# A fused mixing layer with two MLPs, its main loop unrolled: softmax weights in two buffers and a phase earlier, and the leaky layer as a parametric ReLU in place in PSUM

## The reference

```python
w = softmax(weight_gen, axis=-1)             # (2, 4096, 8 heads, 7 taps)
x_pad = concatenate([zeros(6 rows), x])      # causal, per batch
out[s, h] = sum_k w[s, h, k] * x_pad[s + k, h]     # 24 features a head
h = out @ w_in;  g = maximum(0.01 * h, h)    # leaky layer, 192 -> 2048
x2 = g @ w_out                               # 2048 -> 192
h = x2 @ w_in2;  g = where(h > 0, h, exp(minimum(h, 0)) - 1)   # ELU layer
return g @ w_out2
```

## Time and profile before

| | |
|---|---|
| median of the runs | 1238.52 us |
| the profiled execution | 1236.35 us |
| its span, first to last instruction | 1234.6 us |
| TensorE busy (9808 matmuls) | 1156.0 us, 94% |
| VectorE busy | 828.8 us, 67% |
| ScalarE busy | 740.3 us, 60% |
| GpSimd busy | 486.8 us, 39% |
| mean granted TensorE clock | 0.976 |

### The profile page before, as it was taken

The page is one execution under the profiler, slowest core; times in us unless marked ns, Lnnn a source line. Parts: engine busy times, 40 slices in busy tenths (PEclk is TensorE's granted clock), DMA queues, the critical chain, the costliest instruction groups (busy, mean ns, idle before and its releaser), DMA issues.

```text
span 1234.6 us, 24425 instructions
## 1 busy us (share of the span) xinstructions
PE 1156.0 (94%) x9808; PEld 1007.4 (82%) x9808; DVE 828.8 (67%) x817; ACT 740.3 (60%) x846; POOL 486.8 (39%) x411
## 2 busy tenths in 40 slices
PE   7698998989989899898989989899898989989998
PEld 4576887878889888787878889899787878889986
DVE  6969775756757567575765757567575766756564
ACT  3455756656665565656656565565656656565674
POOL 5919054270824609054180723609145180730000
PEclk9999999999999899899999999899899999999999
DMA  6220112010120200212011120200202001110000
GB/s 173 65 84 27 62 40 63 25 57 16 38 61 25 74 13 25 61 34 65 25 40 34 38 61 25 70 14 28 61 25 74 25 21 52 38 25 27 14 27 27
DMA packets 44651, 54.39 MB, mean 44 GB/s; under 512 B 4116, under 2 KB 32914, under 8 KB 44624
## 3 DMA queue, kind: packets, MB, share of 16 engines
q1 hardware_dynamic: 44624, 54.01, 14.5%
HBM read 36.29 MB, written 17.69 MB: 44 GB/s over the span
## 4 chain that ended last, share of the span: by engine, by line
PE 86%; issue 5%; DVE 4%; POOL 4%; ACT 1%; DMA 1%; SPq 0%; POOLq 0%
PE y_a_rows L617 27%; PE hidden L549 27%; PE y_b L610 19%; PE hidden L553 9%; PE hidden L578 4%; DVE hid_lo L1116 1%; POOL mix L323 1%; POOL prod L311 1%; PE hidden L579 1%; DVE act L1086 1%; DMA xw<-in_x_dram 1%; DVE up_b_lo L998 0%; DVE act L1089 0%; POOL prod L336 0%; DVE up_a_lo L988 0%
## 5 line engine op out<-in xcount | busy, mean ns | idle before, releaser
L617 PE MATMUL y_a_rows<-hid_hi,dn 64*128 64x512 f32 x2048 | 577.0, 394 | 0.0
L1116 DVE TENSOR_TENSOR hid_lo<-act,hid_hi 128x1024 fp32r<-128x1024 f32 x255 | 338.5, 1328 | 217.0 <-ACT hid_hi L908 217.0
L610 PE MATMUL y_b<-hid_hi,dn 64*128 64x512 f32 x1024 | 403.3, 394 | 50.4 <-issue 46.5
L610 PE MATMUL y_b<-hid_lo,dn 64*128 64x512 f32 x1024 | 400.3, 391 | 0.0
L617 PEld LDWEIGHTS y_a_rows<-hid_hi,dn 64*128 64x128 f32 x2048 | 339.8, 188 | 26.6
L617 PE MATMUL y_a_rows<-hid_lo,dn 64*128 64x512 f32 x1024 | 355.8, 392 | 0.0
L908 ACT ACTIVATE hid_hi<-act 128x1024 fp32r<-128x1024 f32 x255 | 268.3, 1052 | 1.7 <-DVE act L1089 1.5
L311 POOL TENSOR_TENSOR mix<-xw,wk 128x384 f32<-128x384 f32 x30 | 27.1, 904 | 579.9 <-DVE wk L1026 577.0
L893 ACT ACTIVATE act<-hidden 128x1024 f32<-128x1024 f32 x127 | 130.5, 1027 | 204.4 <-PE hidden L553 162.5
L610 PEld LDWEIGHTS y_b<-hid_hi,dn 64*128 64x128 f32 x1024 | 192.1, 188 | 72.5 <-issue 54.3
L311 POOL TENSOR_TENSOR prod<-xw,wk 128x384 f32<-128x384 f32 x180 | 243.3, 1358 | 9.4
(11 more groups left out here) (105 smaller groups left out, 1109.5 us busy)
## 6 DMA issues: line engine op xcount, KB each, us to landing
xw<-in_x_dram SPq DMA_DIRECT2D x14, 960.0 KB
raw_b<-squares_out SPq DMA_DIRECT2D x60, 96.0 KB, 2.2
out_dram<-staged SPq DMA_DIRECT2D x15, 384.0 KB, 2.3
squares_in<-prod SPq DMA_DIRECT2D x56, 96.0 KB, 4.5
squares_out<-ya SPq DMA_DIRECT2D x15, 256.0 KB, 2.0
raw_a<-squares_in SPq DMA_DIRECT2D x14, 256.0 KB, 2.9
raw_d<-in_moe_w_out_dram SPq DMA_DIRECT2D x8, 384.0 KB, 4.2
raw_a<-in_moe_w_in_dram SPq DMA_DIRECT2D x8, 256.0 KB, 4.1
```

The lines of the kernel that those rows point to most:

```text
L610: return nc.tensor.matmul(y_b[:, :], dn[m][rows, f, P:2 * P], v[rows, s % HB, HALF[i]], start=start, stop=stop)
L617: return nc.tensor.matmul(bank[:, :], dn[m][rows, f, first:first + P], v[rows, s % HB, HALF[i]], start=(f == 0 and n == 0), stop=(f == FT ...
L1116: nc.vector.tensor_tensor(hid_lo[:, s % HB, :], act[:, s % 2, :], hid_hi[:, s % HB, :].bitcast(f32), ALU.subtract).then_inc(s_lo, 1)
```

## The change

1. The hardware loop is gone: all 32 phases are written out for each engine.
2. The softmax weights have two buffers, and the softmax of chunk c+3 is done in the ELU phase of chunk c (`softmax_a` after step 3, `softmax_exp` after step 4, `softmax_b` after step 5), where it was that of chunk c+1 in the leaky phase of chunk c. That is one phase earlier for each chunk. `turn_mix` goes from step 1 to step 2, behind `add_y`, and the leaky input from steps 4 and 5 to 5 and 6.
3. The leaky step is one parametric ReLU on ScalarE, from `hidden` to `hidden`. Rounding reads `hidden` in the same step; VectorE's rest reads `hidden` too, and the maximum on VectorE is gone. The PSUM buffer is given back by the rest (`hid_lo`), no longer by the maximum.
4. At the start, the weight loads wait until the first x has landed; the weights of chunk 1 are loaded before them and its softmax comes earlier; the part of the weight split that GpSimd did goes to VectorE; one weight load is queued behind the load of chunk 2.

```diff
-        wk = sb("wk", [P, J * H, TAPS], f32)
+        wk = [sb(f"wk{n}", [P, J * H, TAPS], f32) for n in (0, 1)]
...
-        DN_POOL = 1
-        UP1_AT = {2: 1, 3: 2}
-        DN1_AT = {1: 3, 2: 4, 3: 6}
+        UP1_AT = {2: 1, 3: 3}
+        DN1_AT = {0: 0, 1: 2, 2: 5, 3: 6}
...
-            with eng.Fori(2, CH - 1) as c:
+            for c in range(2, CH - 2):
                 emit(0, c, phase_mlp1(c), 1, c - 2)
                 emit(1, c - 1, phase_mlp2(c - 1), 0, c)
+            emit(0, CH - 2, phase_mlp1(CH - 2), 1, CH - 4)
+            emit(1, CH - 3, phase_mlp2(CH - 3), 0, CH - 2)
...
+            load_w(1)
             sp.wait_ge(s_x0, 16)
+            sp.wait_ge(s_x, x_arrived(0))
             load_up(0, 0)
             load_up(0, 1)
...
             sp.wait_ge(s_mix, 1)
-            load_w(1)
...
-            load_up(1, 2)
...
             load_chunk(2)
+            load_up(1, 2)
             load_up(1, 3)
...
-            for n in range(DN_POOL):
-                split_down(pool, nc.gpsimd, 0, n)
             mixing(1)
             mixing(2)
-            with pool.Fori(3, CH) as c:
+            for c in range(3, CH):
                 mixing(c)
...
-                    if not (known(ph) and ph == 0 and s < 2):
-
-                        pe.wait_ge(s_g, g - 1)
+                    of_two, c_two = (dm, dc) if s < 2 else (m, c)
+                    if of_two == 0:
+
+                        pe.wait_ge(s_lo, g - 1)
+                    elif of_two == 1:
+
+                        pe.wait_ge(s_g, ST * c_two + (s - 2) % ST + 1)
                     up(m, input_of(m, c), g, s, False)
...
                 if m == 0:
-                    nc.scalar.activation(act[:, s % 2, :], hidden[:, s % 2, :], ACT.Copy, scale=SLOPE).then_inc(s_act, 1)
+                    nc.scalar.activation(hidden[:, s % 2, :], hidden[:, s % 2, :], ACT.Prelu, alpha=SLOPE).then_inc(s_leak, 1)
...
-                nc.scalar.activation(hid_hi[:, s % HB, :], act[:, s % 2, :], ACT.Copy).then_inc(s_hi, 1)
+                nc.scalar.activation(hid_hi[:, s % HB, :], (act if m else hidden)[:, s % 2, :], ACT.Copy).then_inc(s_hi, 1)
...
                     activation(m, c, g, s)
-                    rounding(g - 1, (s - 1) % ST)
-                    if m:
+                    if s == 0 and dm == 1:
+                        rounding(1, dc, g - 1, ST - 1)
+                    if m == 0:
+                        rounding(0, c, g, s)
+                    else:
+                        if s:
+                            rounding(1, c, g - 1, s - 1)
                         exponential(c, s)
...
                     if m == 0:
-                        activation(m, g, s)
-                        rests(g - 1, (s - 1) % ST)
+                        rests(0, g, s)
                     else:
-                        rests(g - 1, (s - 1) % ST)
-                        activation(m, g, s)
-                    if m == 0 and s == 0 and not (known(c) and c in (0, CH - 1)):
-                        softmax_a(c + 1)
-                    if m == 0 and s == 2 and not (known(c) and c in (0, CH - 1)):
-                        softmax_b(c + 1)
-                    if m == 1 and s == 1 and not (known(c) and c >= CH - 2):
+                        if s:
+                            rests(1, g - 1, s - 1)
+                        activation(c, s)
...
+                    if m == 1 and s == 2 and not (known(c) and c >= CH - 2):
                         turn_mix(c + 2)
-                    if m == 1 and s in (4, 5) and not (known(c) and c >= CH - 2):
-                        mlp1_input_lo(c + 2, s - 4)
+                    if m == 1 and s in (5, 6) and not (known(c) and c >= CH - 2):
+                        mlp1_input_lo(c + 2, s - 5)
+                    if m == 1 and s == 3 and not (known(c) and c >= CH - 3):
+                        softmax_a(c + 3)
+                    if m == 1 and s == 5 and not (known(c) and c >= CH - 3):
+                        softmax_b(c + 3)
```

More of the change, by code:

```diff
@@ L259, in x_arrived @@
         def x_arrived(c):
[L261 removed]
+            return 16 * (2 if c == 0 else X_DMAS - 1 + c)
         def run(eng, emit):
@@ L298, in last_columns, with mix_taps @@
             return ap.rearrange("f (q j t) -> f q j t", q=Q, j=J)
-        def mix_taps(eng, ops, j0, j1, done, before, terms):
+        def mix_taps(eng, ops, j0, j1, done, before, terms, weights):
             n = len(terms)
@@ L480, in _ @@
             turn_in(2)
-            with sp.Fori(2, CH - 2) as c:
+            for c in range(2, CH - 2):
                 turn_out(c - 2)
@@ L813, in softmax_exp @@
                 act_e.wait_ge(s_soft, SOFT_STEPS * c + 2)
-                nc.scalar.activation(wk[:, :, :], wk[:, :, :], ACT.Exp).then_inc(s_exp, 1)
+                nc.scalar.activation(wk[c % 2][:, :, :], wk[c % 2][:, :, :], ACT.Exp).then_inc(s_exp, 1)
             def mlp1_input_hi(c, part):
@@ L912, in first_step @@
                     wait_half(act_e, s_up, s_up1, 0, i)
-                    nc.scalar.activation(act[:, 0, HALF[i]], hidden[:, 0, HALF[i]], ACT.Copy, scale=SLOPE).then_inc(signal(s_act, s_act1, i), 1)
-                softmax_exp(1)
+                    nc.scalar.activation(hidden[:, 0, HALF[i]], hidden[:, 0, HALF[i]], ACT.Prelu, alpha=SLOPE).then_inc(signal(s_leak, s_leak1, i), 1)
+                act_e.wait_ge(s_leak1, 1)
+                rounding(0, 0, 0, 0)
                 round_up(0, 2)
@@ L918, in last_step @@
                 s = ST - 1
-                rounding(END - 1, s - 1)
+                rounding(1, CH - 1, END - 1, s - 1)
                 act_e.wait_ge(s_lo, END - 1)
@@ L973, in _ @@
             mlp1_input_hi(0, 1)
-            for n in range(DN_POOL):
-                round_down(0, n)
+            round_down(0, 0)
             run(act_e, phase)
@@ L1106, in last_step, with activation, rests @@
                                             ALU.subtract).then_inc(signal(s_lo, s_lo1, i), 1)
-            def activation(m, g, s):
-                dve.wait_ge(s_act, g + 1)
-                nonlinearity(m, hidden[:, s % 2, :], act[:, s % 2, :], s_g)
-            def rests(g, s):
+            def activation(c, s):
+                dve.wait_ge(s_act, ST * c + s + 1)
+                elu(hidden[:, s % 2, :], act[:, s % 2, :], s_g)
+            def rests(m, g, s):
                 dve.wait_ge(s_hi, g + 1)
-                nc.vector.tensor_tensor(hid_lo[:, s % HB, :], act[:, s % 2, :], hid_hi[:, s % HB, :].bitcast(f32), ALU.subtract).then_inc(s_lo, 1)
+                nc.vector.tensor_tensor(hid_lo[:, s % HB, :], (act if m else hidden)[:, s % 2, :], hid_hi[:, s % HB, :].bitcast(f32), ALU.subtract).then_inc(s_lo, 1)
             def phase(m, c, ph, dm, dc):
@@ L1154, in phase @@
                                 split_up(0, q)
-                        for n in (1, 2, 3):
+                        for n in range(DN_PARTS):
                             if DN1_AT[n] == s:
@@ L1165, in _ @@
             softmax_b(0)
+            softmax_a(1)
             mixing_share()
@@ L1170, in _ @@
             mlp1_input_lo(0, 1)
+            softmax_b(1)
             split_up(0, 1, (1,))
-            softmax_a(1)
             run(dve, phase)
```

84 lines of the change are left out of this document (45 added, 39 removed).

## The result

| | before | changed |
|---|---|---|
| median (lowest to highest) | 1237.50 us (1236.08 to 1239.02, 4 runs) | 1187.57 us (1184.21 to 1189.24, 4 runs) |
| ratio, 95% interval | | 0.9593 (0.9566 to 0.9620) |
| profiled execution, span | 1234.6 us | 1186.27 us, span 1183.6 us |

A forecast was written before the change was run, and what follows sets the result against it. TensorE's order of work was taken as the bound, stalled by 13 gaps. Span 1234.6 - 46.5 - 19.5 - 13 + 1 = 1156.6 us gave a forecast of 1159 us, range 1150 to 1182.

The forecast's parts named there:

- Terms 1 and 2: TensorE's 13 gaps ahead of a down matmul vanish, -46.5 us, and the low clock behind them, -19.5 us.
- Term 3: Unrolling the loop: 0, since TensorE is busy without a break where the loop turns.
- Term 4: Leaky step as one Prelu in PSUM: 128 maxima leave VectorE, 0 where TensorE bounds, gain at the start.
- Term 6: The start: earlier x and second softmax, earlier mixing of chunk 1, fewer maxima; -13 us, bounds 5 and 18.
- Term 5: ELU steps 5 to 7: softmax and input difference behind step 5 just fit; 1 us of stalls allowed.
- A to F: A fits, 0.63; B little slack, 0.22; C clock falls, 0.04; D tables, 0.02; E gap stays, 0.05; F slow Prelu, 0.03.

The follow-up runs named there:

- e4: Kernel before with the mixing result's transpose moved behind the add of the y halves and the squares' readers one step later; 1184.28 us (0.9569).
- e11: Kernel before with e4's order, unrolled, two weight buffers, softmax a phase ahead, operands on multiples of 256 bytes, old leaky step and start; 1185.81 us.
- e18: e5 without x alone on the queues, with GpSimd splitting the first quarter of the down weights and the second softmax late; 1165.18 us.
- e5: Changed kernel with 128 unused bytes per partition behind the weight buffers, so moving operands start on multiples of 256 bytes; 1165.77 us (0.9420).
- e14: e5 with the squares' readers at ELU steps 4 and 5 and the transpose back at step 1, ahead of the add; 1160.42 us.
- e1: Kernel before with its three run-time loops written out and nothing else; 1246.09 us (1.0059).

## Why the prediction was off, step by step

| term | predicted us | measured us of span | from |
|---|---|---|---|
| 1 and 2, gap and clock | -66 | -52.4 | before to e4 |
| 3, unrolling, with the softmax ahead, once the gap is gone | 0 | +0.2 | e4 to e11 |
| 4, leaky step, with the order of the splits | 0 (8.4 of term 6) | -19.4 | e11 to e18 |
| 5, ELU steps | +1 | +5.7 of stalls, inside the above | waits of e5 |
| 6, start, three of its edits | -13 | +0.8 | e18 to e5 |
| TensorE's own pace | no term | +19.8 | e5 to the changed kernel |

The measured steps lead from 1234.6 to 1183.6 us.

**The step that failed** is "A turn without gap and without low clock is 72.78 - 3.58 = 69.20 us, 4.325 us a step, 0.228 us a pair", carried over to the changed kernel as if TensorE's pace were a constant. The diff changes no matmul; it moves their operands by 896 bytes. That is +21.8 us in the medians (e5): without it the kernel takes 1165.77 us, inside the range and 6.8 us above the 1159. In place of the constant 0.228 us a pair the runs show 0.2267 on multiples of 256 bytes and 0.2324 at 128 past them. No rival of mine named it: A to F are all about waits, the clock and ScalarE.

**Terms 1 and 2** had the right mechanism: the add behind the transpose (e4 cures it by order alone) and the late softmax behind that (in e14 the early softmax leaves the transpose 21.8 us to spare), and the clock recovers with the gap. The size was off by 13.6 us, because the gap was subtracted as though nothing lay under it. Up to 0.99 us a turn of late ELU combination came to light, 16.0 us in e4 against 3.0 before.

**Term 3** held once the gaps were gone (+0.2 us, together with the early softmax). On the kernel with its gaps, unrolling cost 8 us (e1), by the clock behind them.

**Term 4** was wrong in size. The spare time at leaky step 2 and the duration of the Prelu (1.03 forecast, 1.009 measured) were right, and steady turns gained 0.48 us. But most of the start's gain turned out to come with the leaky step.

**Term 6** gave nearly the right time, half of it for the wrong reason. The third ELU step's ReLU came at 111.83 us (before 126.48; forecast 113). I gave 7.4 us, up to the first matmul of phase 1, to a mixing that starts 5.1 us earlier and is 2.3 us shorter, and 6.1 us behind it to the maxima. The second part was right: that stretch took 47.1 us in the changed kernel, against 46.9 forecast. Of the first, the matmul came at 64.76 (forecast 66.1). But with the second softmax, x and the split all undone (e18) it still came at 66.41, against 73.50 before, and the ReLU at 112.41. A shorter mixing, 27.1 us in place of 32.4, makes 5.3 of these 7.1 us. The early start, which I had made the larger part, is worth 1.65 us at that matmul and nothing in the time of the kernel.

**Term 5** fits but for the 0.36 us at ELU step 4, 5.7 us in e5 against the 1 us allowed. It is not at steps 5 to 7, where I looked, but behind `take_y` at step 2, which the order before the change had in the same place. In the changed kernel itself, with its slower TensorE, it is 3.4 us in all.

## What to carry to other kernels

An edit that adds or resizes a tile moves the addresses of all that are allocated behind it; when no wait explains a slower stretch, compare the pitch of equal matmuls in both traces before looking further, and put the moving operands back to where they were (here multiples of 256 bytes) before judging the edit. A gap hides the stalls that would stand behind it: what removing it is worth is bounded by the next late producer, so look for who else would be late at that place. Where several edits fall together at one place of the critical path, undo each and all of them. A sum that comes out right does not show that its terms are right.

## What the runs showed of the hardware that I had not expected

The pace of a stream of fp32r matmuls (64 rows, 512 columns, in pairs) changed with where their moving operands start in SBUF: 4.307 us for 19 pairs at multiples of 256 bytes, 4.350, 4.415 and 4.433 at 64, 128 and 192 bytes past, with clock 1.00 and no wait in the record, and mean durations of a matmul of 386, 388, 391 and 392 ns. Aligning only one half of the operands gave back a fifth of the pace lost, and slowed pairs whose own operands were aligned (0.230 to 0.231 us from start to start against 0.227). Unrolling loops of a kernel that stands in gaps made it slower, 1246.09 against 1238.17 us, with a lower mean clock.
